# A one-hot product for the last expert tile, and the next stage's first rows loaded before its scatter

## The reference

```
attn  = softmax(mask(q k^T / 8)) v          # 4 batches, 8 heads, 768 positions, 64 per head; window 128, 4 sinks
x     = attn as (3072 tokens, 512)
moe:    tokens with x @ w_skip > 0 go to the expert e = argmax(x @ w_gate) of 8
        x[token] += gate * (relu(x[token] @ w1[e]) @ w2[e])      # 512 -> 1024 -> 512
out   = (relu(x @ w_in) ** 2) @ w_out       # every token, 512 -> 2048 -> 512
```

## Time and profile before

| | |
|---|---|
| median of three runs | 957.07 us (955.70 to 958.55) |
| the profiled execution | 961.46 us, of which its span is 960.0 us |
| TensorE (PE), products | 928.3 us busy, 97% of the span |
| VectorE (DVE) | 456.0 us, 47% |
| ScalarE (ACT) | 419.8 us, 44% |
| GpSimd (POOL) | 82.4 us, 9% |
| DMA | 100.04 MB, mean 104 GB/s |

### The profile page before, as it was taken

How to read it: one execution, slowest core, us unless ns; L and a number is a source line. 1 busy time by engine, 2 the same in 40 slices (tenths; PEclk the granted TensorE clock), 3 DMA queues, 4 the chain that set the end, 5 groups by cost and what they waited for, 6 DMA issues and landing times.

```text
span 960.0 us, 17066 instructions
## 1 busy us (share of the span) xinstructions
PE 928.3 (97%) x5240; PEld 743.9 (77%) x5241; DVE 456.0 (47%) x1392; ACT 419.8 (44%) x969; POOL 82.4 (9%) x148
## 2 busy tenths in 40 slices
PE   7999999989999999599999999999999999999998
PEld 5778777767888877488888888888888888888886
DVE  5787899785767778343232223222322222222223
ACT  6888999745666677243122123112321222122122
POOL 3112111223111111000000000000000000000000
PEclk9999999989999999799999999999999999999999
DMA  5456774376666687600020002000200020002001
GB/s 179 167 169 207 226 233 149 121 278 215 240 238 223 224 314 256 240 4 1 0 71 19 1 1 87 0 0 0 87 0 0 0 87 0 0 0 87 0 0 44
DMA packets 40291, 100.04 MB, mean 104 GB/s; under 512 B 5821, under 2 KB 5949, under 8 KB 40240
## 3 DMA queue, kind: packets, MB, share of 16 engines
q1 hardware_dynamic: 33936, 83.33, 25.5%
q0 software_dynamic: 6160, 16.02, 4.8%
q10 hardware_dynamic: 144, 0.07, 0.0%
HBM read 78.25 MB, written 25.56 MB: 108 GB/s over the span
## 4 chain that ended last, share of the span: by engine, by line
PE 90%; DVE 3%; DMA 2%; issue 2%; ACT 1%; DVEq 0%; ACTq 0%; SPq 0%; POOLq 0%; POOL 0%
PE bank L1090 28%; PE bank L1104 28%; PE bank L994 7%; PE bank L975 7%; PE bank L834 5%; PE bank L889 4%; PE bank L862 4%; PE bank L900 1%; PE bank L983 1%; DMA w_raw<-in_weights 1%; PE bank L1071 1%; PE bank L914 1%; PE bank L882 1%; PE bank L967 1%; ACT prob L640 0%
## 5 line engine op out<-in xcount | busy, mean ns | idle before, releaser
L1455 DVE TENSOR_TENSOR g<-relu_c 128x512 f32<-128x512 f32 x96 | 66.5, 692 | 364.9 <-ACT relu_c L780 364.8
L780 ACT ACTIVATE relu_c<-bank 128x512 f32<-128x512 f32 x96 | 57.4, 598 | 388.6 <-PE bank L1090 388.6
L1090 PE MATMUL bank<-x_hi,w_lo 128*128 128x512 f32 x384 | 152.6, 398 | 0.8 <-DVE x_lo L1448 0.8
L1104 PE MATMUL bank<-w_hi,g_lo 128*128 128x512 f32 x384 | 153.1, 399 | 0.0
L1090 PE MATMUL bank<-x_lo,w_hi 128*128 128x512 f32 x384 | 152.8, 398 | 0.0
L1090 PE MATMUL bank<-x_hi,w_hi 128*128 128x512 f32 x384 | 152.8, 398 | 0.0
L1104 PE MATMUL bank<-w_hi,g_hi 128*128 128x512 f32 x384 | 152.0, 396 | 0.0
L1104 PE MATMUL bank<-w_lo,g_hi 128*128 128x512 f32 x384 | 151.8, 395 | 0.0
L640 ACT ACTIVATE prob<-score,neg_max 128x264 f32<-128x264 f32 (+1 forms) x192 | 94.0, 496 | 16.6 <-DVE neg_max L1164 16.6
L1430 DVE TENSOR_TENSOR w_lo<-w_raw,w_hi x70 | 82.0, 1221 | 21.2 <-ACT w_hi L748 11.1
L1090 PEld LDWEIGHTS bank<-x_hi,w_lo 128*128 128x128 f32 x384 | 72.6, 189 | 19.0 <-DVE x_lo L1448 1.2
(11 more groups left out here) (141 smaller groups left out, 1285.3 us busy)
## 6 DMA issues: line engine op xcount, KB each, us to landing
w_raw<-in_weights SPq DMA_DIRECT2D x80, 512.0 KB, 5.1
x_c<-x_rows SPq DMA_DIRECT2D x28, 256.0 KB, 3.6
k_in<-in_kT SPq DMA_DIRECT2D x24, 264.0 KB
q_in<-in_qT SPq DMA_DIRECT2D x24, 256.0 KB, 3.1
v_in<-in_v SPq DMA_DIRECT2D x24, 256.0 KB
x_rows<-x_row SPq DMA_DIRECT2D x24, 256.0 KB
out<-w_raw SPq DMA_DIRECT2D x12, 512.0 KB, 2.8
x_res<-routed POOLq DMA_DIRECT2D x16, 260.0 KB, 4.5
```

What stands on the lines that cost most here:

```text
L1090: ins = eng.matmul(hc_ps[f % 2][:, :], w[f // UNIT][:, f % UNIT, wcols], x[:, c, :], start=(c == 0 and n == 0), stop=(c == DC - 1 and n == 2))
L1104: ins = eng.matmul(yc_ps[s][:, :], gg[:, f % 2, s * P:(s + 1) * P], w[f // UNIT][:, f % UNIT, DM:CH], start=(f == 0 and n == 0), stop=(f = ...
L1455: eng.tensor_tensor(g[:, f % 2, :], relu_c[:, f % 2, :], relu_c[:, f % 2, :], ALU.mult).then_inc(s_cg, 1)
```

## The change

SP, in the last expert's loop, stops before the fourth of the eight chunks of unit 9, waits for the scatter of the last tile but one, loads the first 512 rows for the dense stage, and goes on with the chunks. For that its loop over experts is written out, with constant unit numbers. `x_c` is now a view of `x_row`, and `x_row`, `column`, `x_raw` and `x_res` get space of their own that the dense stage doesn't use again otherwise.

The rows so loaded lack what the last tile adds to them. ScalarE and VectorE form the last tile's `gate * y_ps` as a high and a low part, 128 rows by 512. VectorE makes a matrix `sits` of 128 by 512 that has a one where the token number of the row is that of the column (a row of another token number has zeros alone). TensorE transposes the loaded rows into banks 6, 7, 3 and 4, with the accumulation left open, and adds the product of each part with `sits` to each bank, 8 products in all. The last of them in a bank raises `s_cturn`.

GpSimd scatters the last tile as before, but waits for the four loads first; ScalarE's first `g_hi` and VectorE's first `g_lo` wait for that scatter. SP's waits ahead of the dense stage shrink to the one for the last scatter, now ahead of the load of the second 512 rows. GpSimd no longer issues the load of rows and of residuals beyond the last tile, and writes the column numbers once with an iota. `y_of` holds gate and token number.

```diff
 (SP)
-                eng.dma_start(w_raw[:, f, :], weights[bass.ds(u, 1), :, f, :].rearrange("o p d -> (o p) d")).then_inc(s_whead if f < HEAD else s_wtail, 16)
+                eng.dma_start(w_raw[:, f, :], weights[u, :, f, :]).then_inc(s_whead if f < HEAD else s_wtail, 16)
...
                 for f in range(UNIT):
+                    if e == E - 1 and f == HEAD - 1:
+
+                        eng.wait_ge(s_bscatter, tiles * 16)
+                        close(eng)
+                        load_x(0)
                     if f == HEAD - 1 or f == UNIT - 1:
...
-            each_expert(eng, expert)
+            tiles = all_tiles(eng)
+            for e in range(E):
+                first, end = expert_tiles(eng, e)
+                expert(e, e % 2, 0 if e == 0 else first, end)
...
-            eng.wait_ge(s_brows, tiles * 16)
-            close(eng)
             eng.wait_ge(s_bscatter, tiles * 16 + 16)
             close(eng)
-            eng.wait_ge(s_bres, tiles * 16 + 16)
-            load_x(0)
-
             eng.wait_ge(s_cturn, 4)
             load_x(1)
 (GpSimd)
+            eng.iota(column[:, :], [[1, SUPER]], base=0, channel_multiplier=0).then_inc(s_column, 1)
-            with eng.Fori(1, tiles) as n:
+            with eng.Fori(1, tiles - 1) as n:
                 load_rows(n + 2)
                 store_rows(n)
+            eng.wait_ge(s_brow, tiles + 1)
+            close(eng)
+            for n in range(4):
+                eng.wait_ge(s_cx[n], 16)
+            scatter_rows(y_of[:, 1:2], y_row[:, :])
 (ScalarE)
             each_expert(eng, expert)
+            eng.wait_ge(s_brow, tiles + 1)
+            close(eng)
+            eng.activation(part_hi, y_ps[:, :], ACT.Copy, scale=y_of[:, 0:1].bitcast(F32)).then_inc(s_parthi, 1)
...
             def upper(k, f):
                 eng.wait_ge(s_cg, k + 1)
+                if isinstance(k, int) and k == 0:
+                    eng.wait_ge(s_bscatter, tiles * 16 + 16)
+                    close(eng)
 (TensorE)
                 for c in range(DC):
-                    ins = eng.transpose(xT0_ps[c][:, n * P:(n + 1) * P], x_c[:, n, c * P:(c + 1) * P], ident[:, :])
-                    if n == 3:
-                        ins.then_inc(s_cturn, 1)
+                    eng.matmul(xT0_ps[c][:, n * P:(n + 1) * P], x_c[:, n, c * P:(c + 1) * P], ident[:, :], is_transpose=True,
+                               start=(n == 0), stop=False, skip_group_check=True)
+            eng.wait_ge(s_sits, 1)
+            eng.wait_ge(s_parthi, 1)
+            for c in range(DC):
+                eng.matmul(xT0_ps[c][:, :], part_hi[:, c * P:(c + 1) * P], sits, start=False, stop=False, skip_group_check=True)
+            eng.wait_ge(s_partlo, 1)
+            for c in range(DC):
+                eng.matmul(xT0_ps[c][:, :], part_lo[:, c * P:(c + 1) * P], sits, start=False, stop=True, skip_group_check=True).then_inc(s_cturn, 1)
 (VectorE)
             each_expert(eng, expert)
+            eng.wait_ge(s_brow, tiles + 1)
+            close(eng)
+            eng.wait_ge(s_column, 1)
+            eng.tensor_copy(last_token[:, :], y_of[:, 1:2]).then_inc(s_last, 1)
+            eng.wait_ge(s_last, 1)
+            eng.tensor_scalar(sits, column[:, :], last_token[:, 0:1], None, ALU.is_equal).then_inc(s_sits, 1)
+            eng.wait_ge(s_parthi, 1)
+            eng.scalar_tensor_tensor(out=part_lo, in0=y_ps[:, :], scalar=y_of[:, 0:1].bitcast(F32), in1=part_hi.bitcast(F32),
+                                     op0=ALU.mult, op1=ALU.subtract).then_inc(s_partlo, 1)
```

More of the change, by code:

```diff
@@ L122, in sbr @@
             return sb(name, shape, dt, small, "right")
+        x_row = sbr("x_row", [P, XR, ROW], F32)
+        column = sbr("column", [P, SUPER], I32)
+        x_raw = sbr("x_raw", [P, ROW], F32)
+        x_res = sbr("x_res", [P, ROW], F32)
         pad_row = sbr("pad_row", [P, ROW], F32)
@@ L171, in build @@
         y_row = sbr("y_row", [P, DM], F32)
-        y_id = sbr("y_id", [P, 1], I32)
+        y_of = sbr("y_of", [P, 2], I32)
+        last_token = sbr("last_token", [P, 1], F32)
         small.close()
-        x_c = sb("x_c", [P, 4, DM], F32, side="right")
+        kept = sb("kept", [P, XR * ROW + SUPER], F32, side="right")
+        x_c = x_row[:, :, 0:DM]
+        part_hi, part_lo, sits = hb_hi[:, 0, :], hb_lo[:, 0, :], hb_lo[:, 1, :]
         x_hi = sb("x_hi", [P, DC, SUPER], F32R, side="right")
@@ L193, in build @@
         hc_ps, xTc_ps, yc_ps = bank[0:2], bank[2:4], bank[4:8]
-        xT0_ps = bank[2:6]
+        xT0_ps = bank[6], bank[7], bank[3], bank[4]
         s_zero, s_mask, s_ident, s_const = sem("s_zero"), sem("s_mask"), sem("s_ident"), sem("s_const")
@@ L377, in each_expert, with all_tiles @@
                     body(e, slot, first, end)
+        def all_tiles(eng):
+            return eng.value_load(table[0:1, 2 * E - 1:2 * E], min_val=E + 1, max_val=MAX_TILES)
         def expert_tiles(eng, e):
@@ L471, in _, with load_x @@
             eng.dma_start(x_raw[:, :], routed[P:2 * P, :]).then_inc(s_bx, 16)
+            def load_x(m):
+                for n in range(4):
+                    eng.dma_start(x_c[:, n, :], x_rows[bass.ds((m * SUPER) % N + n * P, P), :]).then_inc(s_cx[n], 16)
             def expert(e, slot, first, end):
@@ L615, in _ @@
             eng.wait_ge(s_pad, 16 * (E - 2))
-            tiles = eng.value_load(table[0:1, 2 * E - 1:2 * E], min_val=E + 1, max_val=MAX_TILES)
+            tiles = all_tiles(eng)
             store_rows(0)
-            with eng.Fori(1, tiles) as n:
+            eng.iota(column[:, :], [[1, SUPER]], base=0, channel_multiplier=0).then_inc(s_column, 1)
+            with eng.Fori(1, tiles - 1) as n:
                 load_rows(n + 2)
                 store_rows(n)
+            eng.wait_ge(s_brow, tiles + 1)
+            close(eng)
+            for n in range(4):
+                eng.wait_ge(s_cx[n], 16)
+            scatter_rows(y_of[:, 1:2], y_row[:, :])
         @block.scalar
```

7 lines of the change are left out of this document (2 added, 5 removed).

## The result

The changed kernel takes 948.04 us in the median of four runs (945.66 to 949.08), the kernel before beside it on the same chip 956.38 us. The ratio is 0.9907, with a 95% interval from 0.988 to 0.9934. Faster, then, by 8.3 us in the medians, by 6.3 to 11.5 us by the interval, where the prediction had 11.1 us and a median of 946.0. Two later series with the same kernel gave 0.9896 (0.9875 to 0.9918) and 0.9890 (0.9869 to 0.9911).

The account below looks back on a forecast made before the run. TensorE bounds the kernel except at the seam between expert and dense stages, worth at most 15.9 us. Gap 8.8 plus clock 2.3 gives 11.1 us: 957.07 − 11.1 = 946.0 us, range 943.9 to 949.5.

Parts of the forecast that it names:

- first case: The forecast itself: loads early, clock held at the seam; 946.0 us, 944.4 to 947.5, chance 0.72.
- the rival of late rows: At the seam the last 128 rows land at 393 to 395 us; 946.5 to 948.5 us, chance 0.08.
- the fallen clock: The dense stage starts at half clock again, losing the 2.29 us; 948.3 up to 949.5 us, chance 0.15.
- The seam: Border of expert and dense stages, at 384 to 408 us: gap and low clock, 11.1 us to be gained.
- The gap: TensorE from last expert product to first dense one: 4.8 us instead of 13.6, 8.8 us earlier.
- The one-hot path: Transposes, compare, high and low parts, eight products replace the memory round trip; first dense product at 395.8, not 404.63.
- The clock: TensorE's granted clock taken as held through the seam, 2.29 us more gained in the first dense products.
- The first rival: The clock falls all the same at the seam; 948.3 up to 949.5 us, chance 0.15.
- Last scatter and weights: Scatter lands by 398.8, over 3 us before the first g_hi; weight chunk 3 near 391, 5 us to spare.
- The second, third and fourth rivals: At the seam: rows late, 946.5 to 948.5 (0.08); weights late, over 958 (0.03); loads no earlier, 957 (0.02).

Follow-up runs that it names:

- third profile: The changed kernel, unedited, profiled a third time beside the last version: 947.62 us, ratio 0.9890.
- second profile: The changed kernel, unedited, run and profiled again: 947.99 us against 957.31 for the kernel before.

## Why the prediction was right

**The time.** The median came out at 948.04 us. That lies in the prediction's stated range (943.9 to 949.5), but above the range of its first case alone (944.4 to 947.5), where it also fits the rival of late rows and nearly that of the fallen clock. So the time by itself could not say which case it was; the traces do. The seam gave what was forecast. The forecast for a profiled execution, 950.4 us, came out as 945.66, because the part ahead of the seam, which the change does not shorten by design, was 391.04 − 387.05 = 3.99 us shorter in that execution; the rest of the difference is the 0.8 us behind the seam, named below.

**The gap.** Forecast 4.8, measured 4.79. The scatter of the last tile but one let SP go on 381.37 − 378.33 = 3.04 us after its issue, where 3 were taken (3.05 in the second and third profile). The reason given, that no weight chunks run beside it, holds here: the last scatter, with weight chunks beside it, took 5.7. Four loads and a TensorE that came 5.5 us after their issue left no wait. The late place of the same loads costs 6.84 us of seam; this is the greater part of the change, and shown.

**The one-hot path.** Transposes 1.91 (forecast 1.76), high part 0.69 (0.61), compare 0.49 (0.69 taken, bounds 0.23 and 0.69), low part 0.75 (0.75), from the first high product to the first dense one 391.86 − 389.05 = 2.81 (forecast 395.8 − 393.05 = 2.75). The transposes were priced 0.15 too low and the compare 0.2 too high; TensorE stood 0.26 us between the two (0.15 by the forecast), and the small misses cancel. Leaving the path out gives back 1.97 us.

The Trainium skill (ScalarE: Activation LUTs, What ACT_TABLE_LOAD costs) has some 93 ns for a per-partition scale; 0.69 against 0.60 for a pass of the same shape without one (`h_b`, L726) agrees. The Trainium skill (VectorE: DVE Perf Modes, The perf-mode tier table) lets a pass with one tensor input out of SBUF go at twice the pace of one with two; 486 against 692 ns here bears out the direction. By that the compare's price could have been set under 0.69 beforehand.

**The clock.** Held at 1.00 through the seam, and 36 dense products took 8.67 us (13.48 − 4.81) where they had taken 10.87: 2.2 against the forecast 2.29. Fillers in the kernel before gave the same 2.2 alone. The first rival falls in all three profiles of the changed kernel, and in the four of its variants that load the rows early. But the prediction's ground for it was weak, and in part this was luck. It took a stretch of the expert stage (353 to 358 us) in which TensorE stood "some 2 us in one piece" and kept the clock; the trace has 1.73 us there. At the same place of the program three other profiles, with pauses of 2.75, 2.88 and 3.24 us, lost the clock, and four, with 2.20 to 2.46 us, kept it. One tile later the changed kernel's second profile lost it behind a pause of 2.06 us, where the profile without the one-hot part kept it over 2.15. From another execution the same reading would have given the other answer. In the run with fillers in part of the gap the clock fell with TensorE busy for 3.33 of 6.00 us; in the changed kernel it held from 387 to 392 us with TensorE busy for 4.03 of 5.00. How near that is to a fall no run shows. The Trainium skill (TensorE: Matmul & The Clock Gate, Part 4: PE-mode transpose) says that transposes do not count as busy in the way that products do; no run here separates that from the engine's pauses, and 1.91 us of transposes did not cost the clock.

**Last scatter and weights.** The last scatter is issued at 389.17 and lands 5.7 us later, at 394.9; the first g_hi is at 398.26 with no wait ahead of it. The first conversion of the last unit's weights in the dense stage starts at 392.41, right behind the high parts of x. The second, third and fourth rivals fall by the waits shown above.

**What was mis-sized.** The seam gave 24.46 − 13.48 = 10.98 us, against 11.1. The price of the first rival was added up a little too high: 948.3 and some 1 us more is 949.3, not 949.5. A term that the prediction does not have is some 0.8 us behind the seam (544.50 to 543.67): all traces with the change have it, all without don't. Each later round of the dense stage is shorter by 0.14 us. The first transposes of two rounds, before (91.46 us apart) and after (91.32):

```profile
488.23 0.38 PE L1071 MATMUL bank<-ident,x_c 128*128 128x128 f32 x2
...
579.69 0.38 PE L1071 MATMUL bank<-ident,x_c 128*128 128x128 f32 x2
```

```profile
473.17 0.49 PE L1095 MATMUL bank<-ident,x_row 128*128 128x128 f32 x3
...
564.49 0.38 PE L1095 MATMUL bank<-ident,x_row 128*128 128x128 f32 x2
```

Each round has the same 400 transposes and products and no long pause in either kernel; spread over them the difference is some 0.3 ns each, and the mean step from one start to the next over all that lies behind the seam is 228.55 ns before and 228.22 after. The change also moves buffers; whether that is the cause was not tried.

**What stays open.** By trace the change is worth 10.98 + 0.8 = 11.8 us, by the medians of three comparisons 8.3, 9.3 and 10.8 us, with intervals that reach from 6.3 to 12.6; 11.8 lies inside two of the three. Three things differ ahead of the seam from execution to execution, in both kernels: the attention stage's last score products begin near 180 or near 182 to 183 us, the clock falls or not at 190 to 202, and the 13th tile's second layer comes 14 to 18 us behind the 12th's where most tiles take 12.3. The second can be followed in the clock of the timed runs. Of the 46 runs of the kernel before in the first two series, 18 had a mean granted clock of 0.992 and took 956.5 us in the mean, 16 had 0.989 and took 959.8. Both profiles of 0.989 that run the seam as before (the kernel before, and that with SP's loop written out) have the fall at the passage and the fall at the seam; that 0.992 means the seam's fall alone is inferred, since no profile of the kernel before shows it. Of 16 runs of the changed kernel 13 had 0.994 to 0.996 and took 948.1 us in the mean, and its third profile, with 0.996, has the fall at the passage; two had 1.0 and took 946.0, and its first profile, one of them, has no fall before the last 2 us. Compared like with like, then, the change is worth 959.8 − 948.1 = 11.7 us with the fall at the passage and 956.5 − 946.0 = 10.5 without, the latter from two runs. If the clock is read rightly, most of what the medians lack is the mix: more of the changed kernel's runs have the fall at the passage. Why so many, and whether the change itself makes it more frequent, was not settled; fillers at the passage raised the clock and did not move the time measurably.

## What to carry to other kernels

At the border of two stages, cut the traces at fixed products and compare the piece between them: it came out equal to 0.02 us in three profiles of one kernel whose spans differ by 2.5. A load that depends on almost everything but the last tile can go out early if the last tile's share is added on the fast engine; price the added path on the chain (here 2 us) against the round trip through memory that it replaces (here 10.8 us, from a gap of 13.59 to one of 2.83). Count the clock as a term of its own, with its price from rows at either level (here 2.2 us). Before resting a forecast of the clock on one row, look at the same place in other profiles: here it differed from one execution to the next. And sort timed runs by their granted clock before comparing medians, since two kernels can have different mixes.

## What the runs showed of the hardware that was not expected

- Fillers at full pace for 7.87 us did not keep the clock through the next 5 us of short transposes with pauses (TensorE busy for 3.33 of 6.00 us): it went from 1.00 to 0.50 at about 405.6 us in that trace.
- At the same place of the expert stage the clock fell behind a pause of 2.06 us in one profile and held over one of 2.15 us in another.
- The clock came back during short work: with the rows loaded late it rose to full during the eight one-hot products, behind 3.7 us of transposes at half clock.
- A compare of 512 int32 columns with a value for each partition took 0.49 us on VectorE, less than the two-input pass of 0.69.
- The dense stage behind the seam ran some 0.8 us shorter (544.50 to 543.67) in all eight traces that have the change, some 0.3 ns for each product.
